# A one-row-tile broadcast matmul spread over all 128 rows, and one cast moved behind a copy, in a fused attention and two-layer expert kernel

## The reference

```python
kv = einsum('bhsd,bhse->bhde', k, v)                # q, k, v: 8 images x 8 heads x 576 x 64
out = einsum('bhsd,bhde->bhse', q, kv)              # linear attention
x = out / sqrt(mean(out * out, -1) + 1e-6) * g_norm # RMS norm of each head
h = sigmoid(x @ w_gate) * (x @ w_val) @ w_out       # 4608 tokens, 512 -> 1536 -> 512
y = h @ w_in                                        # 512 -> 2048
g = y where y >= 1, 0 where y <= -1, else (y + 1) ** 2 / 4
result = g @ w_out2                                 # 2048 -> 512
```

## Time and profile before

| | |
|---|---|
| three timed runs | 1667.20, 1667.77, 1670.38 us (median 1667.77) |
| the profiled execution | 1663.86 us, span 1662.1 us |
| PE / PEld busy | 99% / 97% |
| DVE / ACT / POOL busy | 73% / 53% / 12% |
| granted TensorE clock | 1.00 of full speed |
| DMA | 278.91 MB, mean 168 GB/s |

### The profile page before, as it was taken

The page is one execution under the profiler, slowest core; times in us unless marked ns, Lnnn a source line. Parts: engine busy times, 40 slices in busy tenths (PEclk is TensorE's granted clock), DMA queues, the critical chain, the costliest instruction groups (busy, mean ns, idle before and its releaser), DMA issues. The chain is left out here.

```text
span 1662.1 us, 31802 instructions
## 1 busy us (share of the span) xinstructions
PE 1645.1 (99%) x12471; PEld 1616.1 (97%) x12471; DVE 1217.0 (73%) x1733; ACT 885.3 (53%) x1612; POOL 195.8 (12%) x258
## 2 busy tenths in 40 slices
PE   8999999999999999999999999999999999999999
PEld 5899999999999999999999999999999999999999
DVE  5666777777877675876778887777777687766664
ACT  5666666655555554544445655555555444444442
POOL 2300001014432220100002400000001200000000
PEclk9999999999999999999999999999999999999999
DMA  7534444334776778745344433333438964444450
GB/s 269 179 125 144 132 148 142 114 130 133 253 250 232 245 241 288 248 157 155 117 143 140 165 129 143 118 118 136 167 143 267 341 185 135 129 128 127 128 137 29
DMA packets 229317, 278.91 MB, mean 168 GB/s; under 512 B 33072, under 2 KB 172848, under 8 KB 229168
## 3 DMA queue, kind: packets, MB, share of 16 engines
q1 hardware_dynamic: 217104, 233.35, 42.4%
q0 software_dynamic: 12064, 43.52, 8.2%
HBM read 156.76 MB, written 120.06 MB: 167 GB/s over the span
## 5 line engine op out<-in xcount | busy, mean ns | idle before, releaser
L1584 PE MATMUL x<-t_hi,v_lo 128*128 128x288 f32 x1664 | 495.8, 298 | 2.4 <-DVE v_lo L1104 0.9
L1585 PE MATMUL x<-t_lo,v_hi 128*128 128x288 f32 x1664 | 491.2, 295 | 0.0
L1586 PE MATMUL x<-t_hi,v_hi 128*128 128x288 f32 x1664 | 489.8, 294 | 0.0
L1584 PEld LDWEIGHTS x<-t_hi,v_lo 128*128 128x128 f32 x1664 | 312.0, 188 | 7.2 <-issue 2.1
L1586 PEld LDWEIGHTS x<-t_hi,v_hi 128*128 128x128 f32 x1664 | 313.3, 188 | 0.0
L1585 PEld LDWEIGHTS x<-t_lo,v_hi 128*128 128x128 f32 x1664 | 312.5, 188 | 0.1
L1584 PE MATMUL y<-t_hi,v_lo 128*128 128x288 f32 x832 | 248.2, 298 | 0.5 <-DVE c L1107 0.2
L1585 PE MATMUL y<-t_lo,v_hi 128*128 128x288 f32 x832 | 245.6, 295 | 0.0
L1586 PE MATMUL y<-t_hi,v_hi 128*128 128x288 f32 x832 | 245.0, 294 | 0.0
L1584 PE MATMUL x<-v_hi,t_lo 128*128 128x256 f32 x576 | 163.3, 283 | 2.7 <-ACT o_kept L1070 2.5
L1585 PE MATMUL x<-v_lo,t_hi 128*128 128x256 f32 x576 | 163.1, 283 | 0.0
(11 more groups left out here) (187 smaller groups left out, 3505.7 us busy)
## 6 DMA issues: line engine op xcount, KB each, us to landing
g_scratch<-c_tile SPq DMA_DIRECT2D x128, 288.0 KB, 2.4
gq<-g_scratch SPq DMA_DIRECT2D x64, 512.0 KB, 6.2
h_scratch<-gate SPq DMA_DIRECT2D x192, 144.0 KB, 2.0
hq<-h_scratch SPq DMA_DIRECT2D x32, 864.0 KB, 5.1
stage<-w_in POOLq DMA_DIRECT2D x68, 256.0 KB, 3.8
kv_ring<-kv_in SPq DMA_DIRECT2D x30, 512.0 KB, 4.4
fold_hi<-v_hi SPq DMA_DIRECT2D x14, 896.0 KB, 5.4
fold_lo<-v_lo SPq DMA_DIRECT2D x14, 896.0 KB, 6.9
```

Source lines behind the costliest of these rows:

```text
L1584: nc.tensor.matmul(dst, s_lo, m_hi, start=start, stop=False, skip_group_check=True)
L1585: nc.tensor.matmul(dst, s_hi, m_lo, start=False, stop=False, skip_group_check=True)
L1586: return nc.tensor.matmul(dst, s_hi, m_hi, start=False, stop=stop, skip_group_check=True)
```

## The change

It makes the spread's weights and its moving tile 128 rows tall. The rows beyond 48 are zeros: the 0/1 matrix is built and cast on all 128 rows, and `inv_pair` (128 x 288) is set to zero once by POOL, among the constants. Per image only rows 0 to 47 of `inv_pair` are written, as before. In D, ACT does item 4 no longer ahead of the list but behind the copy of the first product of unit 0, ahead of item 5.

```diff
-CONSTANTS = 7 + 2 * (P // D)
+CONSTANTS = 8 + 2 * (P // D)
...
-            ones = flat(kept[:])[0:PAIR, 0:2 * H * D]
+            ones = flat(kept[:])[:, 0:2 * H * D]
             make(nc.gpsimd.memset(ones, 0.0))
+            make(nc.gpsimd.memset(inv_pair[:].bitcast(f32), 0.0))
...
-            nc.scalar.copy(spread_r[0:PAIR, :], flat(kept[:])[0:PAIR, 0:2 * H * D]).then_inc(spread_const, 1)
+            nc.scalar.copy(spread_r[:], flat(kept[:])[:, 0:2 * H * D]).then_inc(spread_const, 1)
...
-            for e in range(3, D_SLOTS):
-                split_d_item(e)
+            split_d_item(3)
...
+                if p == 0:
+                    split_d_item(4)
                 if p + D_SLOTS < len(SEQ):
                     split_d_item(p + D_SLOTS)
...
-                    ones = spread_r[0:PAIR, N * h + P * c:N * h + P * (c + 1)]
-                    nc.tensor.matmul(banks[h][:, 0:C], ones, inv_pair[0:PAIR, :], start=True, stop=True).then_inc(spread_done, 1)
+                    ones = spread_r[:, N * h + P * c:N * h + P * (c + 1)]
+                    nc.tensor.matmul(banks[h][:, 0:C], ones, inv_pair[:], start=True, stop=True).then_inc(spread_done, 1)
```

## The result

The changed kernel takes 1658.74 us (median of six runs, 1656.14 to 1662.79), the kernel before 1668.28 us beside it (six runs, 1667.20 to 1670.47). The ratio is 0.9942, 95% interval 0.9927 to 0.9958: faster by 9.5 us. The forecast was 1659.7 us, 8.1 us of gain.

What follows compares the result with a forecast made beforehand. TensorE, busy 99% of the span, was taken as the bound. Spread pairs gave 7.7 + 0.4 = 8.1 us, with c = 3 pairs, constants and D at 0: 1667.8 - 8.1 = 1659.7 us, range 1656 to 1664.5.

Steps and rivals of the forecast that it cites:

- 20 pairs x 0.385 us: Spread pairs of images 1 to 7 between products, waiting for nothing: stops both ways go, 7.7 us gained.
- 2 x 0.19: First spread pairs of images 1 and 7, which wait for DVE's inverse: only the way out gained, 0.4 us.
- 0 for the six c = 3: Last spread pairs of images 1 to 6, before the 64-row chunk: net 0, bounds 0 to 1.2 us gain.
- the moved stop: At the six c = 3 pairs: the stop ahead goes, one of 0.19 us comes between pair and 64-row chunk.
- Nothing of it is given back: Behind the spread pairs TensorE stays the bound, so the 8.1 us gained there is kept.
- Constants at 0: Start: POOL's new memset adds 0.45 us, selects stay at 2.42, hidden by idle time; price 0, upper bound 1.8 us.
- D at 0: Start of D: the 2.6 us stall for ACT's copy goes, but later waits take it back; bounds 0 and 2.5.
- the first two waits: Start of D: new TensorE waits for DVE's low parts of item 4, 0.7 us, and item 5, 1.7 us.
- The third step: Start of D: the last half load, behind a full DMA queue, takes back the remaining 0.25 us; wait 0.6 us.
- The range: Whole kernel, 1656 to 1664.5 us: low end half of D and c = 3; high end half the gain plus run spread.

Runs made afterwards that it cites:

- e3: Changed kernel with the spread's matmuls taking only rows 0 to 63 of the 128 zero-padded ones; 1667.90 us (one run).
- e5: Changed kernel with the spread's matmuls taking only rows 0 to 95 of the 128 zero-padded ones; 1657.59 us (one run).
- e1: Changed kernel with item 4 in D back at its old place, so only the spread is changed; 1657.93 us, ratio 0.9944 to the kernel before.
- e0: Changed kernel measured again without any edit; 1657.15 us, ratio 0.9940 to the kernel before.
- e9: Changed kernel with kv chunks of 128, 128, 128, 96, 96 rows and DVE's low part of item 5 early; 1656.11 us, ratio 0.9935.
- e2: Kernel before with only the move of item 4's cast in D, spread still on 48 rows; 1667.61 us, ratio 0.9997.
- e6: Changed kernel with DVE making the low part of item 5 ahead of two of its sums in D; 1658.62 us, ratio 0.9944.
- e7: Kernel of e6 without the low parts of the last four half loads of D (2 MB less); 1657.34 us, ratio 0.9935.
- e4: Changed kernel with kv chunks of 128, 128, 128, 96, 96 rows instead of four of 128 and one of 64; 1656.98 us, ratio 0.9939.
- e10: Kernel of e6 run once more for another profile; 1660.48 us (one run).
- e11: Kernel of e1 run once more, item 4 at its old place; 1656.68 us (one run).

## Why the prediction was right

- **20 pairs x 0.385 us, 2 x 0.19, and 0 for the six c = 3.** Right, and the sum too: 8.1 to 8.3 us in the trace for 8.1. The five starts around a pair take 1.05 or 1.06 us before and 0.65 to 0.67 after, in each of the 20 places. e3 and e5 show the cause by changing the rows alone, and the 64-row chunk shows the moved stop.
- **Nothing of it is given back.** Right: e1 and e0 keep it to the end. Stage B takes 268.1 us in every profile and stage C 359.5 to 360.2, whatever the spreads, and what differs up to B differs among kernels with the same spreads.
- **Constants at 0.** Right: 0.41 us for the 0.45 forecast, hidden behind the wait for the first inputs (e9), and POOL's work goes by columns.
- **D at 0.** Right in the sum (e2: 0.9997) and in the first two waits, 0.80 to 0.93 and 1.67 us for 0.7 and 1.7. The third step was stated too firmly. I put a wait of 0.6 us for the last half load and called it a limit that takes back whatever is left; without the edits of e6 it was 0, 0, 0.19 and 1.36 us. DVE's order alone takes back nearly all of the lead, the full DMA queue only what is left behind it.
- **The measured gain is 9.5 to 10.2 us, the traced one 8.1 to 8.3.** Part of it is the clock, which the forecast left out. Most executions of either kernel have a granted clock a little under 1.000, and each 0.001 goes with some 1.7 us. The profiles under 1.000 show where it goes, to stretches at 0.5, the 1.2 GHz level: 3.4 us in e3 and e7 (0.999), which loses 1.7 us, and 6.8 us in the changed kernel's first profile, e4, e6 and e10 (0.998). In that first profile they lie in the start (12.5 to 15.9 and 33.0 to 36.4 us), beginning 1.8 and 1.3 us behind the end of a wait for inputs, of 1.68 and 2.13 us. Between executions with 1.000 the distance of the kernels is smaller than the measured gain: the kernel before, e2 and e3 have 9 such executions with a mean of 1665.1 us; changed, e0, e1, e5 and e11 have 10, with 1657.3 us. That is 7.8 us. At 0.999 it is 21 executions with 1666.8 us and six with 1658.2, 8.7 us. The rest is that the kernels with spreads of more than 64 rows had 1.000 more often, 10 of 20 times against 9 of 51. Whether the change has a hand in that, or chance alone, was not tried.
- **The range.** 1656 to 1664.5 us holds the measured 1658.74, but its low end was worked out wrongly: half of D and half of the c = 3 pairs below 1659.7 would be 1657.8 us; 1656 is all of both (2.5 and 1.2 us).

## What to carry to other kernels

Look at the distance from one matmul start to the next where the shape changes, not at durations: a small matmul between large ones can cost more in the two changes than in itself. Where its contraction is short and its operands stay in place, pad them with zeros once to the height of its neighbours; 96 rows were enough here and 64 were not, and the padding cost columns of one memset, not rows. Before paying for a stall's removal, work out what the same engine waits for next, with the times at which each of these things is ready: in D two such lines of arithmetic gave the result before it was run.

## What the runs showed of the hardware that was not expected

- 96 rows go at the pace of 128, without a stop, while 64 and 48 rows stop both ways (e3, e4, e5). The weights' 48 columns in the mean squares never did. The Trainium skill, "TensorEngine Tiling (Array Packing)", section "Key Properties", says that changing the tiling mode drains TensorE; under "Available Configurations" it lists 64 rows and 64 columns alike as modes. For rows the trace agrees that a change costs something, some 0.19 us each way, though 96 rows, which are in no mode of that list, went at the pace of 128. For columns no such cost is seen at 48. Whether any matmul here is in a mode of its own in the page's sense, and whether the stop is that drain, no run shows.
- A late sum in D costs twice. In e3, e4, e6 and e10 the sum for item 4 came 2.2 to 2.9 us later, as the store of C's last tiles ahead of it took longer (in e10 9.19 us, against 7.06 in e2). TensorE then stood for 3.0 to 3.7 us in one piece. Before the wait it had run without a gap at 1.00; in the last 0.5 to 1.5 us of the wait the granted clock fell to 0.5 of full speed, the 1.2 GHz level, and stayed there for 3.4 us (e3) or 6.8 us (the others) in all. In the ten other profiles, whose longest wait in the start of D is 2.65 us, the clock did not fall there. The chain and the table of stretches in e10:

```profile
1282.36 9.19 DMA g_scratch<-c_tile
1291.57 5.88 DMA gq<-g_scratch
```

```profile
1296.00:1300.00 4.00, 1.68 (x15) 1.47 (x13) 1.36 (x2) 1.22 (x2) 2.27 (x5) 0.96 0.83 246
1300.00:1304.00 4.00, 2.77 (x13) 2.80 (x14) 4.00 (x4) 1.04 (x2) 3.20 (x7) 0.50 1.07 303
1304.00:1308.00 4.00, 4.00 (x26) 4.00 (x26) 4.00 (x5) 3.47 (x6) 0.87 (x2) 0.69 1.11 392
```

  The start of D is then 51 to 52 us in place of 48.6. Less its waits it is 46.0 to 46.2 us in the ten other profiles, 47.3 in e3 and 48.3 to 48.7 in e4, e6 and e10: so the low clock costs 1.2 us in the one and 2.2 to 2.6 us in the others. This late sum was seen in 4 of 11 profiles with the move of item 4 and in none of 3 without. The late store lies ahead of all that the move touches, so it should strike both; that is argued, and three profiles are too few to show it.
